# Attention and two MLPs on one core: an unused 32-byte tensor behind the constants moves the start of 27 buffers

## The reference, cut to what matters

```python
scores = scale * np.matmul(q, k.transpose(0, 1, 3, 2))          # 4 x 8 heads, 576 x 576, head_dim 64
thresh = np.max(scores, axis=-1, keepdims=True) - tau
scores = np.where(scores >= thresh, scores, -1000000000.0)
scores = scores - np.max(scores, axis=-1, keepdims=True)
attn = np.exp(scores)
attn = attn / (np.sum(attn, axis=-1, keepdims=True) + 1e-09)
x = np.matmul(attn, v)                                          # regrouped to 2304 x 512
...
h = x @ w_in                       # first MLP: 512 -> 2048
r = np.maximum(h, 0.0)
x = (s * (r * r) + b) @ w_out      # 2048 -> 512
...
h = x @ w_in                       # second MLP, same sizes
out = (np.maximum(h, 0.0) + alpha * np.minimum(h, 0.0)) @ w_out
```

## Time and profile before

| | us |
|---|---|
| three runs, median | 1102.38 |
| three runs, lowest and highest | 1101.58 and 1102.41 |
| the profiled execution, its own time | 1102.66 |
| its span, from the first instruction to the last | 1100.8 |
| attention, to the first `up` matmul | 293 |
| MLPs, to the last matmul | 803 |

### The profile page before, as it was taken

One profiled execution on the slowest core, in us unless ns is written; L12 is line 12 of the kernel. 1 busy time (PEld: TensorE's weight loads), 2 busy tenths in 40 slices (PEclk: granted clock), 3 DMA queues, 4 the chain that ended last, 5 costly groups with the idle time before them and its releaser, 6 DMA issues.

```text
span 1100.8 us, 18966 instructions
## 1 busy us (share of the span) xinstructions
PE 1085.6 (99%) x5826; PEld 889.5 (81%) x5826; DVE 531.3 (48%) x1016; ACT 507.8 (46%) x946; POOL 257.6 (23%) x438
## 2 busy tenths in 40 slices
PE   7999999999999999999999999999999999999998
PEld 6777777777688888888888889888888888888897
DVE  7998989999543332242242246522422332332232
ACT  4877878787654332232232235544433333333343
POOL 3665656566564200000000014322000000000000
PEclk9999999999999999999999999999999999999999
DMA  8666666665011100000000003311100100010010
GB/s 189 160 155 143 155 142 150 148 150 140 20 60 49 46 1 1 1 0 0 0 0 0 0 20 88 86 48 29 39 0 0 38 0 0 0 38 0 0 39 20
DMA packets 86554, 59.28 MB, mean 54 GB/s; under 512 B 49376, under 2 KB 69872, under 8 KB 86512
## 3 DMA queue, kind: packets, MB, share of 16 engines
q1 hardware_dynamic: 83248, 57.58, 20.5%
q10 hardware_dynamic: 3264, 1.18, 0.5%
HBM read 30.94 MB, written 4.72 MB: 32 GB/s over the span
## 4 chain that ended last, share of the span: by engine, by line
PE 90%; ACT 3%; DVE 2%; SPq 2%; issue 2%; DMA 0%; POOL 0%; ACTq 0%; POOLq 0%; DVEq 0%
PE psum L940 23%; PE psum L938 23%; PE psum L939 23%; PE psum L1072 6%; PE psum L1038 5%; PE psum L967 3%; PE psum L969 3%; DVE act_r L874 2%; PE psum L1067 1%; SPq L427 1%; PE psum L951 1%; ACT pt L638 1%; PE psum L1046 1%; ACT win_hi L593 1%; ACT ex L616 1%
## 5 line engine op out<-in xcount | busy, mean ns | idle before, releaser
L940 PE MATMUL psum<-x_hi,win_lo 128*128 128x512 f32 (+1 forms) x640 | 238.7, 373 | 0.0
L939 PE MATMUL psum<-x_lo,win_hi 128*128 128x512 f32 (+1 forms) x640 | 238.2, 372 | 0.0
L938 PE MATMUL psum<-x_hi,win_hi 128*128 128x512 f32 (+1 forms) x640 | 238.1, 372 | 0.0
L939 PEld LDWEIGHTS psum<-x_lo,win_hi 128*128 128x128 f32 x640 | 120.2, 188 | 24.0
L938 PEld LDWEIGHTS psum<-x_hi,win_hi 128*128 128x128 f32 x640 | 120.3, 188 | 23.0 <-DVE x_lo L867 0.2
L940 PEld LDWEIGHTS psum<-x_hi,win_lo 128*128 128x128 f32 x640 | 120.2, 188 | 23.0
L885 DVE SCALAR_TENSOR_TENSOR act_r<-act_n,nalpha,act_r 128x512 f32<-128x512 f32 (+1 forms) x80 | 56.2, 702 | 160.0 <-ACT act_r L717 159.8
L874 DVE SCALAR_TENSOR_TENSOR act_r<-act_r,s_c 128x512 f32<-128x512 f32 (+1 forms) x80 | 72.4, 905 | 116.4 <-ACT act_r L706 116.4
L709 ACT ACTIVATE g_hi<-act_r,b_c 128x512 fp32r<-128x512 f32 (+1 forms) x80 | 54.5, 682 | 152.5 <-PE psum L940 122.4
L550 POOL TENSOR_SCALAR ex<-ex,none_in,rinv 128x576 f32<-128x576 f32 x142 | 117.1, 826 | 32.2 <-DVE rinv L807 31.0
L877 DVE SCALAR_TENSOR_TENSOR g_lo<-act_r,b_c,g_hi 128x512 fp32r<-128x512 f32 (+1 forms) x80 | 56.3, 704 | 133.6 <-ACT g_hi L709 133.6
(11 more groups left out here) (93 smaller groups left out, 1613.2 us busy)
## 6 DMA issues: line engine op xcount, KB each, us to landing
k_twice<-k_hi SPq DMA_DIRECT2D x64, 144.0 KB, 2.5
stage<-in_moe_w_out_dram SPq DMA_DIRECT2D x32, 256.0 KB, 2.6
out_dram<-stage SPq DMA_DIRECT2D x18, 256.0 KB, 2.2
q_both<-q_hi SPq DMA_DIRECT2D x32, 128.0 KB, 2.3
q_both<-q_lo SPq DMA_DIRECT2D x32, 128.0 KB, 2.3
win_raw<-in_moe_w_in_dram SPq DMA_DIRECT2D x16, 256.0 KB, 3.1
stage<-in_moe_w_in_dram SPq DMA_DIRECT2D x16, 256.0 KB, 2.7
raw_q<-in_q_dram SPq DMA_DIRECT2D x30, 128.0 KB, 2.4
```

The source lines that it names most:

```text
L938: nc.tensor.matmul(dst, lhs[0], rhs[0], start=first, stop=False)
L939: nc.tensor.matmul(dst, lhs[0], rhs[1], start=False, stop=False)
L940: return nc.tensor.matmul(dst, lhs[1], rhs[0], start=False, stop=final)
```

## The change

One tensor is allocated behind the last constant and never used: no instruction reads or writes it.

```diff
         nalpha = sb("nalpha", [P, FC])
         one_exp = sb("one_exp", [P, 1])
+        sb("to_line", [P, 8])
```

## The result

| | before | changed |
|---|---|---|
| median of 4 runs, us | 1102.27 | 1091.36 |
| lowest and highest, us | 1101.58 and 1102.41 | 1091.03 and 1091.91 |
| ratio, 95% interval | | 0.9899 (0.9887 to 0.9911) |
| profiled execution, us; its span | 1102.66; 1100.8 | 1091.03; 1089.1 |

The change makes the kernel 10.9 us faster. I had forecast 53 us; 1091 was the time of my first rival.

The account below looks back on a forecast made before the run. PE was taken to bound the kernel, by the distance between matmul starts. MLPs 50.2 us plus attention 3, other engines and DMAs 0, gave 53.2 us off 1102.66: 1049 us, range 1043 to 1104 (1043 to 1065 for the line forecast alone).

Parts of the forecast that it names:

- first rival: MLPs: only the relation of the two operands' starts matters; `up` falls to 226.7 ns, attention unchanged, 1091 us; chance 0.20.
- What bounds the kernel: Whole kernel: PE is busy nearly all the time, so only matmul start distances or a rare gap can move the MLPs.
- So addresses seem to matter to PE, through both operands.: MLPs: `up` (weights at 0, moving at 96) costs 233 ns, `down` 227.5; the step shows before the first `win_hi` weights.
- The price of the MLPs: PE in the MLPs: `up` saves 26.1 us, `down` 18.8, 256-column `up` 3.4 and `down1` 1.9; sum 50.2 us.
- the line count: Float32r moving operands: 128-byte lines, 17 touched in place of 16 at 512 columns, 226.7 ns; nothing left over on a line.
- a rival: Whole kernel: the change does nothing, as PE may read in units of 16 or 32 bytes; 1102 us; chance 0.18.
- The attention, 3 us: 592 score matmuls in the attention save at most 10 ns each, 5.9 us; half taken, 3 us, bounds 0 and 5.9.
- The rival on the slow side: `down` and scores: weights at remainder 0 are dear; `down` rises to 233 ns, +9.0 us, scores +1, 1112 us; chance 0.15.
- The page's rule: Warm matmuls: N columns at 2.4 GHz plus about 2.5 ns, 215.7 ns for bf16 at N=512; MLP sum would be about 51 us.
- The page on memory: SBUF cachelines of 16 bytes, with two hits per line asked for; by that rule the change does nothing.

Follow-up runs that it names:

- both32: Changed kernel plus 32 bytes ahead of win_hi, `to_line` kept, so all matmul operands start at remainder 32 by 128; 1091.32 us.
- rel96_moving0: Changed kernel with 32 bytes ahead of win_hi and no `to_line`: win_hi and win_lo at remainder 32, other operands at 0; 1102.76 us.
- third probe: Changed kernel plus 48 groups of 24 equal float32r matmuls, moving operand shifted 0 to 240 bytes against weights; 226.7 to 234.6 ns at 512 columns.
- line160: Changed kernel with `to_line` of 160 bytes in place of 32, so every buffer behind it begins 128 bytes further; 1104.66 us.
- g32: Changed kernel with 32 bytes between wout_lo and g_hi, which moves g_hi, g_lo, act_r and act_n to 32; 1104.53 us.
- the probe: Changed kernel plus 29 groups of 24 equal matmuls behind its last one, with operand starts, widths and types varied; 226.7 ns with nothing moved.
- rest64: Changed kernel with `to_line` of 96 bytes, so the moving operand of `up` is 64 bytes ahead of its weights; 1094.68 us.
- last192: Changed kernel with moving operands of the last, 256-token tile 192 bytes further (second MLP's `up`, and `down1`); 1091.26 us.

## Why the prediction was wrong

- *What bounds the kernel.* Right. PE's rate was the whole story, the other engines had room, and their times did not change with 32 bytes more (within 1.4%). That holds for the MLPs' blocks; at the change of layers PE waits for VectorE, as forecast.
- *"So addresses seem to matter to PE, through both operands."* Right, and the one sentence that should have led. The trace held a clean comparison, `up` at 233 and `down` at 227, and the interval at which the step shows pointed at the weights.
- *The price of the MLPs: the failed step.* "I take the upper end, because the line count reproduces 226.7 and 133.3 ns without a free constant." It was chosen from two fits (and a third at 120.0). But all moving float32r operands of the trace had one remainder, so that "one line more" and "32 cycles more for any float32r matmul" gave the same numbers at every width. They could not be told apart, and the changed kernel has 226.7 and 120.0 with everything on a multiple of 128. `down` saved its edge intervals alone, 1.4 us and not 18.8; `up` 9.4 and not 26.1; the last tiles lost 0.2 and did not save 5.3. What the runs showed in place of lines is the distance of the two operands: both32, with every start off a line of 128 bytes, takes 1091.3 us, and rel96_moving0, with the moving operand on one, 1102.8.
- *The evidence against it.* I had the row that spoke against whole lines: `up` at 256 columns took 118.3 ns, less than nine lines' 120.0. It stood under a rival. It should have cost the forecast more than it did.
- *The attention, 3 us.* Too much. The scores kept 133.3 ns and nothing was gained. By the same mechanism there was nothing to gain: both operands of each score matmul moved by the same 32 bytes, so their distance stayed. Even another distance would have mattered little, since at 288 columns the third probe has 130.4 to 134.2 ns.
- *The first rival* named mechanism, place and size: 1536 x 6.3 + 1 us, 1091. The median is 1091.36; its parts are 9.4 + 1.4 - 0.2 us. What it did not have is the measure: by 256 bytes, not by 128. The change met that by chance, because `win_hi` and `to_line`'s end both have the remainder 128 by 256.
- *The rival on the slow side* (weights at remainder 0 are dear) is refuted by both32 and the change; the slow side does exist by the same mechanism as the gain, in line160 and g32, 1104.5 us.
- *The page's rule.* The Trainium skill's spacing for warm matmuls (TensorE: Matmul & The Clock Gate, "Step-by-step: what each phase is for") is met by bfloat16 and, per record, by float32 in the probe, 2.5 ns above their columns. The float32r streams did not meet it: 13.3 ns above the columns at 512 even in the best state.
- *The page on memory* in the Trainium skill (SBUF — State Buffer, "Specifications (TRN2)", 16-byte cachelines) would have had no change, by my reading of it. This kernel's 10.9 us disagree with what I drew from it.

What stays open: why the two reads meet with a period of 256 bytes, what the 32 cycles are that remain at 512 columns, and why at 256 columns half of them go at certain distances. With 32 weight columns they do not shrink, and with float32 and bfloat16 there is only 2.5 ns. Open too is why some distances disturb the blocks behind them (32 and 128 bytes) and another that is as slow does not (224).

## What to carry to other kernels

Where TensorE bounds a kernel with float32r matmuls of 512 columns, give the weights and the moving operand the same start by 256 bytes, and check it in the built addresses: a small tensor allocated in between shifts everything behind it, and costs or gives back 1%. At 256 columns the map is another, and a rate from a probe of equal matmuls has to be tried in the kernel. Look at the distances between starts, not at busy time, and compare the matmuls of one width with each other; two rates for one shape are a lead. When a constant fits several rows, ask whether any row varies what the theory says it depends on; if none does, the fit has chosen nothing.

## What was unexpected of the hardware

- Two streams of PE that are each in order disturb each other by where they start: 226.7 to 234.6 ns at 512 columns over 16 distances, with nothing else running.
- The disturbance can outlast its cause. In line160 and in g32's first MLP the blocks with equal starts that follow a slow block need about seven matmuls to return to 226.7 ns (2.76 us per block against 2.72), which made those kernels slower than the one before by 2.5 and 2.1 us. Behind slow blocks at a distance of 224 bytes it is only the first interval (2.73 us). A change of width does it too, with all starts equal: in the changed kernel's last tile the six `down2` matmuls of a block, 512 columns each, behind `up` of 256 take 1.39 us, 231 ns each.
- At 256 columns one and the same distance has more than one rate. At 64 bytes it was 117.5 ns in a probe of 24 equal matmuls and 113.3 in rest64, between blocks at distance 0; at 192 bytes 113.8 in the probe, 114.9 in last192's `down1` and 117.8 in its second `up`.
